# Three dense matmuls ahead of each level of the first stage of a recurrent-attention and MLP kernel

## The chip, the cores and the metric

One core of a Trainium2 chip runs the kernel. The metric is the device time of one execution in microseconds; the lower the better. Before the change it is 1013.24 us, the median of three runs (1012.25 to 1013.42).

## The reference

Everything is float32. A linear recurrence over 768 steps (4 batches, 8 heads, 48 channels a head) is followed by an RMS norm, a gated MLP (384 to 1536 to 384) and a squared-ReLU MLP (384 to 2048 to 384), over 3072 tokens.

```python
for t in range(S):
    cur = einsum('bhd,bhe->bhde', u[None] * k[t], v[t])
    y[t] = einsum('bhd,bhde->bhe', r[t], state + cur)
    state = w[t][..., None] * state + einsum('bhd,bhe->bhde', k[t], v[t])
xn = y / sqrt(mean(y * y) + 1e-6) * rms_g
x = (silu(xn @ w_gate) * (xn @ w_val)) @ w_out
out = (s * relu(x @ w_in) ** 2 + b) @ w_out2
```

## The kernel before

The 3072 tokens are worked in six stages (`NSB`) of 512. A stage is two blocks (`blk` 0 and 1) of 256 tokens. The first program block, `attention_and_gated_phase`, does the recurrence and the gated MLP; a second one does the squared MLP. From stage 1 on, the recurrence of stage s is interleaved with the gated MLP of stage s-1, so that TensorE always has 512-column matmuls beside the small ones. Stage 0 has nothing to be interleaved with: `first_attention` does it alone, and only then does the first gate matmul (L609) start.

The recurrence is done by doubling. At level l (0 to 6) the queries R in the second half of each pair of 2^l tokens are matched against the keys K. `level(s, l, blk)` issues 32 float32 matmuls on a 64 x 64 quarter of the array each, 32 columns wide, which the trace shows as 64 weight loads and 64 matmuls (L481). When they are done, VectorE multiplies K by the decays of that level (L923), copies the tile under a mask from PSUM to `near` (`place`, L940, levels 0 to 4) and doubles the decays (L915); GpSimd multiplies R by the decays (L1189). The next level of the same block waits for K and R. Level 5 is placed by ScalarE (L734), level 6 is `top_level` (L499), placed by ScalarE too (L752). In what follows (l, blk) is a level of stage 0.

Stage 0 runs by the list `FIRST_ORDER`: (0,0), (1,0), (0,1), (2,0), (1,1), (3,0), (2,1), (4,0), (3,1), (5,0), (4,1), (6,0), (5,1), (6,1). All engines follow their own program in order. The tiles of stage 0 are two banks each (the program's names in brackets): block 0 alternates between `level_ps` and `mix_gate_ps`, block 1 between `o01_ps` (o_ps in the trace) and `value_o2_ps` (value_o_ps), by whether l is even or odd. So a level must wait, in `level_out`, for level l-2 of its own block to be placed.

TensorE also runs matmuls whose results nobody reads. `run_up(15)` does 15 of 128 x 128 x 128 on a tile of ones (`y_sb[0]`) at the start. `keep_busy(n, ps)` does n of the same shape on the identity; it stands ahead of level (4,1), after (6,0), (5,1) and (6,1), and at some later places. Each such float32 matmul shows as two weight loads and two matmuls.

SyncE issues the loads of stage 0 by what TensorE has finished: three pieces of the gated weights (`w_raw`, 384 KB each) after (0,1), keys and queries by token after (1,0) and (1,1), values and one weight piece each after (2,0) and (2,1), the sixth weight piece after (3,1). ScalarE copies the first six weight pieces (`upper_weights`, L785) in order, each when it has landed, before it places level (5,0); level (6,0) waits for that placement.

Of the kernel before, what the change touches and what calls it, by code (L numbers as in the profile page):

```python
# [14 lines left out]
P = 128  # L15
# [10 lines left out]
NEAR = LV - 2  # L26
# [25 lines left out]
def wait(eng, sem, value):  # L52

    if not isinstance(value, int) or value > 0:
        eng.wait_ge(sem, value)
# [58 lines left out]
def placed(s, l, blk):  # L114

    return FIRST_PLACED.index((l, blk)) + 1 if s == 0 else 2 * NEAR + (NEAR - 1) * (s - 1) + l


def copied(s, blk):

    return 2 * (blk + 1) if s == 0 else 2 * (s + 2)
# [22 lines left out]
def attention_and_gated_phase(nc, block, a, whole, first, x1_dram, y_dram, x1_out, x_hi, x_lo, const_in_squared, level_ps, mix_gate_ps,  # L144
# [38 lines left out]
    with ExitStack() as ctx:  # L183
        def sb(name, shape, dt=F32):
            return ctx.enter_context(nc.sbuf_tensor(name, shape, dt, side="right"))
# [10 lines left out]
        y_sb = [sb(f"y{i}", [P, DM]) for i in range(CH)]  # L196
# [49 lines left out]
    def level_tile(s, l, blk):  # L246

        if s > 0:
            return pairs_ps(s, blk)[:, :, blk * HALF:(blk + 1) * HALF]
        ps = ((level_ps, mix_gate_ps), (o01_ps, value_o2_ps))[blk][l % 2]  # L250
        return ps[:].rearrange("p (j t) -> p j t", t=SUB)[:, :, 0:HALF]
# [42 lines left out]
    def level_out(eng, s, l, blk):  # L294

        if l < 0:
            return
        if l < NEAR:
            wait(eng, cp_done, placed(s, l, blk))
        else:  # L300
            wait(eng, near_done, copied(s, blk))

    def keys_ready(eng, s, l, blk):
        if l == 0:
            eng.wait_ge(k_in[blk], (s + 1) * 16)
        else:
            wait(eng, kmul_done, level_no(s, l - 1, blk))

    def queries_ready(eng, s, l, blk):
        if l == 0:  # L310
            eng.wait_ge(r_in[blk], (s + 1) * 16)
        else:
            wait(eng, rmul_done, level_no(s, l - 1, blk))
# [15 lines left out]
    def halves(ap, l):  # L329

        return ap.rearrange("p (n two m) -> p n two m", two=2, m=1 << l)
# [131 lines left out]

    @block.tensor
    def _(pe):
        def level(s, l, blk):
            if s == 0:
                level_out(pe, s, l - 2, blk)
            elif l > 1:
                level_out(pe, s, l - 1, blk)  # L470
            if s > 0 and l == 1:
                wait(pe, yo_done, CH * s)
            keys_ready(pe, s, l, blk)
            queries_ready(pe, s, l, blk)
            keys = HALF if l == NEAR else SUB
            for q in range(Q):
                for i in range(2):
                    for h in range(2):
                        rows = slice(h * SUB, (h + 1) * SUB)
                        first_key = q * P + i * SUB  # L480
                        mm = pe.matmul(level_tile(s, l, blk)[i * SUB:i * SUB + keys, h * Q + q],  # L481
                                       K[blk][rows, first_key:first_key + keys],
                                       halves(R[blk][rows, first_key:first_key + SUB], l)[:, :, 1],
                                       start=True, stop=True, skip_group_check=True)
            mm.then_inc(level_done, 1)
# [155 lines left out]
        def attention(s, k):  # L641
            if k in LEVEL_AT:
                for blk in range(2):
                    level(s, LEVEL_AT.index(k) + 1, blk)
            if k == TOP_AT:
                for blk in range(2):
                    top_level(s, blk)
            if k == 20:
                turn_keys(s, 0)
                turn_keys(s, 1)  # L650
                turn_keys(s, 2)
            if k == 22:
                turn_keys(s, 3)
                update(s, 0)
                update(s, 1)
            if k == 24:
                update(s, 2)
                update(s, 3)
                attend(s, 0)
            if k == 26:  # L660
                attend(s, 1)
# [7 lines left out]
        def first_attention():  # L669

            run_up(15)
            for l, blk in FIRST_ORDER:
                if l == LV - 1:
                    top_level(0, blk)
                    level_out(pe, 0, NEAR - 2 if blk == 0 else NEAR, 1)
                    keep_busy(2, value_ps)
                else:
                    level(0, l, blk)
                if l == NEAR - 1 and blk == 0:
                    pe.wait_ge(eye_in, 16)  # L680
                if (l, blk) == (NEAR, 0):
                    level_out(pe, 0, NEAR - 3, 1)
                    keep_busy(1, o01_ps)
                if (l, blk) == (NEAR, 1):
                    level_out(pe, 0, NEAR, 0)
                    keep_busy(1, mix_ps)
                if (l, blk) == (NEAR, 1):
                    turn_keys(0, 0)
                    turn_keys(0, 1)
# [893 lines left out]
```

## Time and profile before

| What | Value |
|---|---|
| median of 3 runs | 1013.24 us |
| the profiled execution's own time | 1013.42 us |
| its span, first to last instruction | 1011.3 us |
| mean granted TensorE clock | 0.985 of full |
| TensorE matmul busy | 994.9 us (98%) |
| VectorE busy | 537.8 us (53%) |
| ScalarE busy | 323.6 us (32%) |
| GpSimd busy | 268.5 us (27%) |
| first gate matmul (end of stage 0's recurrence) | starts at 60.06 us |

Times in the trace are counted from the first instruction, so the execution's own time is 2.1 us more than the span. A matmul counts as busy from its start to a modelled end, so matmuls that follow each other closely overlap in the rows: the start of the next group says more than the length of one. The granted clock has two levels, 1.00 for 2.4 GHz and 0.50 for 1.2 GHz.

### The profile page before, as it was taken

The numbers are of one execution on the slowest core, as the hardware profiler recorded it, in microseconds if no ns is written. First come the engines' busy times: TensorE is split into PE (matmuls) and PEld (weight loads), VectorE is DVE, ScalarE is ACT, GpSimd is POOL, SyncE is SP. The second block draws the span as 40 slices with busy tenths as digits, with TensorE's granted clock in tenths as the row PEclk, the third lists the DMA queues.
The fourth block names the chain that finished last, engine by engine and source line by source line (L and its number), as shares of the span: only waits on it lengthen the run. The fifth ranks groups of instructions, "written<-read, shape, count | busy, mean of one in ns | idle before, by whom it ended". The sixth has DMA issues, their size and how long they took to land.

```text
span 1011.3 us, 24572 instructions
## 1 busy us (share of the span) xinstructions
PE 994.9 (98%) x10584; PEld 862.9 (85%) x10584; DVE 537.8 (53%) x723; ACT 323.6 (32%) x550; POOL 268.5 (27%) x189
## 2 busy tenths in 40 slices
PE   7889999999999999999999999999999999999998
PEld 6878888888888888888888888998998989989898
DVE  6799857764676577557743225506226054161440
ACT  1442323233222313231323445406235053161340
POOL 4655723552463166216700650000000000000000
PEclk7799999999999999999999999999999999999999
DMA  7380252116013501440126201010010010100000
GB/s 273 118 327 5 90 165 93 49 51 217 33 49 111 188 3 52 155 141 3 48 61 232 69 16 64 9 39 16 16 48 0 23 39 8 54 0 16 16 8 23
DMA packets 41980, 73.99 MB, mean 73 GB/s; under 512 B 19105, under 2 KB 26273, under 8 KB 40609
## 3 DMA queue, kind: packets, MB, share of 16 engines
q1 hardware_dynamic: 41312, 71.52, 20.9%
q8 instruction: 73, 1.20, 0.5%
q10 hardware_dynamic: 576, 1.13, 0.3%
q14 instruction: 19, 0.15, 0.0%
HBM read 59.27 MB, written 13.37 MB: 72 GB/s over the span
## 4 chain that ended last, share of the span: by engine, by line
PE 87%; DVE 1%; issue 0%; ACT 0%; DVEq 0%
PE value_o_ps L609 13%; PE mix_gate_ps L609 13%; PE o_ps L1404 10%; PE level_ps L47 10%; PE o_ps L621 9%; PE mix_gate_ps L1404 5%; PE value_o_ps L1404 5%; PE mix_gate_ps L47 5%; PE value_o_ps L47 5%; PE value_o_ps L621 4%; PE level_ps L481 4%; PE mix_gate_ps L557 2%; PE level_ps L557 2%; PE level_ps L535 1%; PE level_ps L499 0%; PE level_ps L519 0%
## 5 line engine op out<-in xcount | busy, mean ns | idle before, releaser
L1478 DVE SCALAR_TENSOR_TENSOR sqr<-relu,sb_col 128x512 f32<-128x512 f32 x96 | 72.3, 753 | 216.9 <-ACT relu L1436 216.9
L1189 POOL TENSOR_TENSOR R<-R,arena 128x512 f32<-128x512 f32 x72 | 117.5, 1649 | 187.2 <-PE level_ps L481 161.9
L1057 DVE TENSOR_TENSOR u_raw<-value_o_ps,u_raw 128x512 f32<-128x512 f32 x66 | 45.5, 689 | 110.8 <-PE value_o_ps L609 110.8
L806 ACT ACTIVATE u_raw<-mix_gate_ps 128x512 f32<-128x512 f32 x72 | 43.1, 598 | 182.8 <-PE mix_gate_ps L609 182.7
L813 ACT ACTIVATE u_hi<-u_raw 128x512 fp32r<-128x512 f32 x66 | 41.7, 631 | 152.3 <-DVE u_raw L1057 152.3
L609 PE MATMUL value_o_ps<-x_hi,w_hi 128*128 128x512 f32 x216 | 85.1, 394 | 0.0
L609 PE MATMUL mix_gate_ps<-x_hi,w_hi 128*128 128x512 f32 x216 | 84.7, 392 | 0.0
L609 PE MATMUL value_o_ps<-x_hi,w_lo 128*128 128x512 f32 x216 | 84.1, 389 | 0.0
L609 PE MATMUL mix_gate_ps<-x_hi,w_lo 128*128 128x512 f32 x216 | 84.1, 389 | 0.0
L609 PE MATMUL mix_gate_ps<-x_lo,w_hi 128*128 128x512 f32 x216 | 84.1, 389 | 0.0
L609 PE MATMUL value_o_ps<-x_lo,w_hi 128*128 128x512 f32 x216 | 84.1, 389 | 0.0
L923 DVE TENSOR_TENSOR K<-K,arena 128x512 f32<-128x512 f32 x72 | 70.2, 989 | 22.3 <-PE level_ps L481 12.8
L1065 DVE TENSOR_TENSOR u_lo<-u_raw,u_hi 128x512 fp32r<-128x512 f32 x66 | 73.0, 1106 | 12.5 <-ACT u_hi L813 12.1
L1483 DVE SCALAR_TENSOR_TENSOR g_lo<-sqr,sb_col,g_hi 128x512 fp32r<-128x512 f32 x96 | 71.5, 745 | 0.8
L1427 ACT ACTIVATE g_hi<-sqr,sb_col 128x512 fp32r<-128x512 f32 x96 | 68.8, 716 | 1.3 <-DVE sqr L1478 1.3
L1404 PE MATMUL o_ps<-wt_hi,g_hi 128*128 128x384 f32 x192 | 64.1, 334 | 0.0
L1404 PE MATMUL o_ps<-wt_lo,g_hi 128*128 128x384 f32 x192 | 64.1, 334 | 0.0
L1404 PE MATMUL o_ps<-wt_hi,g_lo 128*128 128x384 f32 x192 | 64.1, 334 | 0.0
L621 PE MATMUL o_ps<-u_hi,wo_hi 128*128 128x512 f32 x144 | 60.3, 419 | 0.0
L481 PEld LDWEIGHTS level_ps<-R,K 64*64 64x64 f32 (+1 forms) x3392 | 50.1, 133 | 8.9 <-issue 8.8
L621 PE MATMUL o_ps<-u_hi,wo_lo 128*128 128x512 f32 x144 | 56.5, 392 | 0.0
L621 PE MATMUL o_ps<-u_lo,wo_hi 128*128 128x512 f32 x144 | 56.4, 392 | 0.0
(190 smaller groups left out, 2309.4 us busy)
## 6 DMA issues: line engine op xcount, KB each, us to landing
kr_nat<-kr SPq DMA_DIRECT2D x10, 1152.0 KB, 5.7
K<-kT SPq DMA_DIRECT2D x12, 512.0 KB, 4.5
arena<-wT SPq DMA_DIRECT2D x12, 512.0 KB, 6.4
R<-rT SPq DMA_DIRECT2D x10, 512.0 KB, 4.2
w_raw<-wgv SPq DMA_DIRECT2D x12, 384.0 KB, 5.2
v_sb<-v SPq DMA_DIRECT2D x12, 384.0 KB, 4.1
x_scratch<-x_sb SPq DMA_DIRECT2D x18, 256.0 KB, 2.3
x_raw<-x_scratch SPq DMA_DIRECT2D x6, 768.0 KB, 4.3
```

The lines of the kernel that those rows point to most:

```text
L47: mm = pe.matmul(ps, w[:, cols], x[:, k], start=(k == 0 and w is win_hi and x is x_hi), stop=(k == KT - 1 and w is win_lo))
L481: mm = pe.matmul(level_tile(s, l, blk)[i * SUB:i * SUB + keys, h * Q + q], K[blk][rows, first_key:first_key + keys], halves(R[blk][rows, f ...
L609: mm = pe.matmul(ps[:], w[:, f, j, k], x[:, k], start=(k == 0 and w is w_hi and x is x_hi), stop=(k == KT - 1 and w is w_lo))
L621: mm = pe.matmul(o_ps[j][:], w[:, f, j * P:(j + 1) * P], x[:, f % 2], start=(f == 0 and w is wo_hi and x is u_hi), stop=(f == F1 - 1 and w ...
L923: dve.tensor_tensor(k, k, decay(blk, l, 1), ALU.mult).then_inc(kmul_done, 1)
L1057: dve.tensor_tensor(u[:, f % 2], value_ps[:], u[:, f % 2], ALU.mult).then_inc(u_done, 1)
L1065: dve.tensor_tensor(u_lo[:, f % 2], u[:, f % 2], u_hi[:, f % 2].bitcast(F32), ALU.subtract).then_inc(ulo_done, 1)
L1189: pool.tensor_tensor(q, q, decay(blk, l, 0), ALU.mult).then_inc(rmul_done, 1)
L1404: mm = pe.matmul(o_ps[t][:, 0:DM], g[:, f, t * P:(t + 1) * P], w[:, f], start=(f == 0 and g is g_hi and w is wt[0]), stop=(f == F2 - 1 and ...
L1427: act.activation(g_hi[:, f], sq[f % 2][:], ACT.Identity, bias=sb_col[:, 1:2]).then_inc(ghi_done[0], 1)
L1478: dve.scalar_tensor_tensor(out=sq[f % 2][:], in0=relu[f % 2][:], scalar=sb_col[:, 0:1], in1=relu[f % 2][:], op0=ALU.mult, op1=ALU.mult).th ...
L1483: dve.scalar_tensor_tensor(out=g_lo[:, f], in0=sq[f % 2][:], scalar=sb_col[:, 1:2], in1=g_hi[:, f].bitcast(F32), op0=ALU.add, op1=ALU.subt ...
```

## The change

`level` calls a new helper for levels 1 to 4 of both blocks of stage 0 (eight calls), after the wait for the tile to be free and ahead of the waits for keys and queries. The helper issues three matmuls of ones, 128 x 128 x 128, into the first 128 columns of the tile that the level writes next. The level's own matmuls overwrite those columns.

```diff
     @block.tensor
     def _(pe):
+        def stay_warm(ps):
+
+            for _ in range(3):
+                pe.matmul(ps[:, 0:P], y_sb[0][:, 0:P], y_sb[0][:, 0:P], start=True, stop=True, skip_group_check=True)
+
         def level(s, l, blk):
             if s == 0:
                 level_out(pe, s, l - 2, blk)
+                if 0 < l < NEAR:
+                    stay_warm(((level_ps, mix_gate_ps), (o01_ps, value_o2_ps))[blk][l % 2])
             elif l > 1:
                 level_out(pe, s, l - 1, blk)
```

## Rows read from the trace of the kernel before

**Rows 1.** The page: busy time of the engines, and the granted clock in 40 slices.
```profile
PE 994.9 (98%) x10584; PEld 862.9 (85%) x10584; DVE 537.8 (53%) x723; ACT 323.6 (32%) x550; POOL 268.5 (27%) x189
...
PEclk7799999999999999999999999999999999999999
```
**Rows 2.** Stretches: length, busy PE, PEld, DVE, ACT, POOL, clock, DMA share, GB/s.
```profile
6.50:12.00 5.50, 2.33 (x130) 2.08 (x128) 3.11 (x4) 0.00 (x0) 2.47 (x2) 1.00 0.84 315
12.10:20.50 8.40, 7.54 (x256) 7.20 (x256) 7.83 (x10) 1.89 (x3) 6.04 (x4) 0.50 0.65 213
...
34.10:39.30 5.20, 5.18 (x109) 4.78 (x110) 2.65 (x6) 2.63 (x5) 3.27 (x3) 0.50 0.49 151
...
60.00:300.00 240.00, 239.12 (x3593) 198.07 (x3593) 177.94 (x227) 68.94 (x117) 110.56 (x73) 1.00 0.30 104
```
**Rows 3.** Waits of TensorE, whole span: total us, times, longest.
```profile
PE mix_gate_ps L481 <- POOL R L1189: 2.4, 1, 2.4
...
PE o_ps L481 <- issue: 2.0, 2, 1.7
PE level_ps L499 <- ACT near L734: 1.7, 1, 1.7
```
**Rows 4.** Timeline of TensorE: start us, length us, then the idle time before in brackets.
```profile
10.11 1.14 PE L481 MATMUL mix_gate_ps<-R,K 64*64 64x32 f32 x64 [2.42 <-POOL R L1189]
12.04 1.93 PE L481 MATMUL o_ps<-R,K 64*64 64x32 f32 x64 [0.80 <-DMA R<-rT]
13.85 1.93 PE L481 MATMUL level_ps<-R,K 64*64 64x32 f32 x64
...
24.21 0.31 PE L481 MATMUL o_ps<-R,K 64*64 64x32 f32 x1 [1.67 <-issue]
...
26.62 1.93 PE L481 MATMUL value_o_ps<-R,K 64*64 64x32 f32 x64 [0.28 <-POOL R L1189]
...
34.12 1.13 PE L499 MATMUL level_ps<-R,K 64*64 64x64 f32 x32 [1.65 <-ACT near L734]
35.18 1.22 PE L639 MATMUL value_o_ps<-eye 128*128 128x128 f32 x4
36.33 1.08 PE L481 MATMUL value_o_ps<-R,K 64*32 64x32 f32 x64
...
37.92 1.75 PE L519 MATMUL mix_gate_ps<-eye,K 128*128 128x128 f32 x8
39.60 0.69 PE L499 MATMUL o_ps<-R,K 64*64 64x64 f32 x32
...
44.68 1.16 PE L639 MATMUL value_o_ps<-eye 128*128 128x128 f32 x8
```
**Rows 5.** Timeline of VectorE: the key multiplies of (2,0), (1,1) and (3,0).
```profile
16.66 1.64 DVE L923 TENSOR_TENSOR K<-K,arena 128x512 f32<-128x512 f32 x1
...
19.84 0.68 DVE L923 TENSOR_TENSOR K<-K,arena 128x512 f32<-128x512 f32 x1
...
21.91 0.68 DVE L923 TENSOR_TENSOR K<-K,arena 128x512 f32<-128x512 f32 x1
```
**Rows 6.** Timeline of GpSimd's query multiplies: (2,1) and (4,0); then (5,1).
```profile
24.80 2.78 POOL L1189 TENSOR_TENSOR R<-R,arena 128x512 f32<-128x512 f32 x2 [3.18 <-PE o_ps L481]
...
37.61 1.57 POOL L1189 TENSOR_TENSOR R<-R,arena 128x512 f32<-128x512 f32 x1 [0.60 <-PE value_o_ps L481]
```
**Rows 7.** Timelines of SyncE's queue and of ScalarE around the sixth weight piece.
```profile
28.60 4.24 SPq L388 DMA_DIRECT2D w_raw<-wgv  x3
...
32.13 0.84 ACT L785 ACTIVATE w_hi<-w_raw 128x768 fp32r<-128x768 f32 x1 [1.61 <-DMA w_raw<-wgv]
32.88 1.18 ACT L734 ACTIVATE near<-mix_gate_ps 32x512 f32<-32x512 f32 x2
```
**Rows 8.** DMA queues in 14.5 to 15.0 and 21.75 to 22.0: packets, MB, share.
```profile
q8 instruction: 1, 0.02, 19.0%
...
q8 instruction: 1, 0.02, 23.7%
```

## The prediction

> **What bounds the kernel now.** I read the page first, then the stretches, then TensorE's waits, then the timelines of the first 60 us. The page says that TensorE is busy for 98% of the span, with the clock below full only in the first two of 40 slices [rows 1]. From 60 us on the stretches show TensorE busy for 239.12 of 240.00 us at full clock [rows 2]; nothing of the change lies there, so that whatever moves the first gate matmul (60.06 us) moves the end by as much. All that is at stake is stage 0's recurrence.
>
> There TensorE is busy too, but slow: it has the full clock in 6.5 to 12.0 us and half of it in 12.1 to 39.3 us [rows 2]. A level's 64 matmuls take 1.14 us at 2.4 GHz and 1.93 us at 1.2 GHz [rows 4]. Ahead of the fall TensorE had idled 2.42 us for R, done one level, and idled 0.80 us for a load [rows 4]. Ahead of the rise it did level (5,1), one `keep_busy` matmul and eight full-width transposes back to back from 37.92 us [rows 4]. So the quarter-array levels did not bring the clock back in 27 us, although they keep the busy column nearly full (7.54 of 8.40 us); full-width work did.
>
> A faster TensorE is worth only what the waits leave. Four things stand behind it:
> - VectorE, busy 7.83 of 8.40 us in 12.1 to 20.5 us [rows 2]. The key multiply of (2,0) starts at 16.66 us, though that level ended at 13.85 + 1.93 = 15.78 us; those of (1,1) and (3,0), at 19.84 and 21.91 us, have no idle time before them either [rows 4, 5]. Up to 23 us VectorE is some 0.9 us or more behind TensorE and sets the pace.
> - A gap of 1.67 us before the last matmul of (2,1), at 24.21 us, put down to issue [rows 3, 4]. VectorE and GpSimd then wait too: GpSimd idles 3.18 us [rows 6]. At 21.75 us the instruction queue moved one block of 16 KB (0.02 MB) [rows 8].
> - The chain from (3,1), whose end is 26.62 + 1.93 = 28.55 us: SyncE issues the sixth weight piece at 28.60 us, it has landed at 32.13 us, ScalarE copies it for 0.84 us, places (5,0) for 1.18 us, and only then does (6,0) start, at 34.12 us, after TensorE has idled 1.65 us [rows 4, 7]. This is 5.57 us in which TensorE's clock does not matter.
> - From 34.12 to 39.60 us TensorE sets the pace at half clock [rows 2, 4].
>
> **The change, part by part.** It removes nothing, adds no wait and moves no DMA directly. It adds 8 x 3 = 24 matmuls, 48 weight loads and 48 matmul records. Price at 1.2 GHz: eight full-width records from 37.92 to 39.60 us are 0.21 us each; the four of `keep_busy` from 35.18 to the next start at 36.33 us are 0.29 us each, the change to small tiles included [rows 4]. A set of six records costs 1.26 to 1.73 us; I take 1.5. At 2.4 GHz: eight in 1.16 us, 0.145 each, is the dear end [rows 4], half of 0.21 the cheap one: 0.63 to 0.87 us a set; I take 0.8, near the row measured at that clock. A full level and its set are then 1.03 + 0.8 = 1.8 us at full clock, about what the level alone costs now (starts 12.04 and 13.85 us: 1.81 us). That is the whole bargain: with the clock up the sets are paid by the faster levels, with the clock low they come on top.
>
> *The set ahead of (1,0)* falls in the idle 2.42 us before 10.11 us [rows 4] and costs nothing. If that cover were gone it would cost 0.8 us. It ends near 8.4 us, so that TensorE idles again before (1,0) and before (0,1); I expect the clock to fall at about 12 us all the same.
>
> *The set ahead of (2,0)* is therefore run at low clock and delays (2,0) by about 1.5 us, to an end near 16.6 us if the clock rises during it. VectorE takes up that level at 16.66 us anyway [rows 5]. Cost 0; without that cover, 0.8 to 1.7 us.
>
> *The sets ahead of (1,1), (3,0), (2,1)*, at full clock: (1,1) ends near 18.4 us and (3,0) near 20.4 us; VectorE takes them at 19.84 and 21.91 us [rows 5]. Cost 0, gain 0: here the change buys nothing, because VectorE is late. If they ran at low clock, they would cost 1.5 us each less that lag.
>
> *The gap at 24.21 us.* One block of instructions was moved at 14.5 and the next at 21.75 us [rows 8], and two levels are 2 x 128 records, so a block holds about two levels. The five sets up to (2,1) put 60 records ahead of the place where TensorE ran out, so that the same block is needed about half a level earlier, and is asked for earlier, ahead of the 768 KB load that SyncE issues after (1,1). The DMA engines are 0.65 busy in 12.1 to 20.5 us [rows 2]. The bounds: the gap stays as it is (0), or goes (-1.7 us). I take the middle, -0.9 us, since nothing in the trace says which. The Trainium skill, page "Runtime: NRT & Kernel Launch", section "Instruction fetch mechanics", says that blocks are 16 KiB or 256 instructions and that crossing into a new one is mostly hidden. The trace disagrees with "hidden" here, with 1.67 us of idle; by that rule the gap would be something else and would stay, and the sum below would be -0.8 instead of -1.7 us.
>
> *The sets ahead of (4,0) and (3,1).* (3,1) waits for R of (2,1), which GpSimd begins at 24.80 us, right after (2,1), and needs some 1.4 us for [rows 6]; (4,0) and the set ahead of (3,1) fit into that at full clock (1.1 + 0.8 us) but for a few tenths. Faster level against set: 0 (bounds -0.3 and +0.6 us). At low clock they cost 1.5 us each.
>
> *The sixth weight piece* then comes as much earlier as (3,1) ends, 0.9 us; *the set ahead of (4,1)* lies in the 1.65 us of idle before (6,0) and is free [rows 4].
>
> *The tail, 34.12 to 39.60 us.* With the clock up, (6,0), two `keep_busy` matmuls, (5,1) and the transposes would take half of 5.5 us, but (6,1) needs R of (5,1), and GpSimd has to do that of (6,0) first, 1.57 us each [rows 6]: 34.8 + 2 x 1.57 + 0.4 for the hand-overs = 38.3 us against 39.60, a gain of 1.3 us. If the idle before (6,0) lets the clock fall first, it is nothing. I take -0.8 us, the larger part, since the added set fills some of the idle.
>
> Sum: 0 + 0 + 0 - 0.9 + 0 - 0.8 = -1.7 us against the profiled execution's 1013.42 us: 1011.7 us. That execution lies 0.2 us above the median of 1013.24 us, so against the median I say 1011.5 us.
>
> **The rivals.**
> *The clock stays low (slower).* For it: six sets cannot help before the clock has risen, a third to a half of TensorE's time would still be quarter-array levels, and the 0.85 us of `keep_busy` beside (6,0) did not raise it [rows 4]. Against it: the transposes at 37.92 us did, after 1.4 us of themselves and one more matmul [rows 4], and a set of 1.3 us every 3.3 us is nearer to that. The price: from 12.04 us TensorE sets the pace, seven levels at 1.81 us spacing and six sets of 1.5 us: (3,1) ends at 12.04 + 6 x 1.81 + 1.93 + 9.0 = 33.8 us instead of 28.55 us. That is +5.3 us (3.8 to 6.7 for sets of 1.26 to 1.73 us), and the weight piece hands it on: 1018.5 us. It decides if the clock is still low at about 19 us; from there VectorE's lag is used up.
>
> *The clock rises and falls again.* The gap near 22 to 24 us is idle after two rather sparse levels. If the clock falls there, the sets ahead of (4,0) and (3,1) cost 1.5 us each, with about 1 us of it hidden: +2 us, 1015.2 us. For it: at 12 us it fell after such a pattern. Against it: the sets thin the idle out.
>
> *The clock rises and all moves.* The gap goes whole and the clock holds to the end of the tail: -1.7 - 1.3 = -3.0 us, 1010.2 us. The DMA engines speak against it: 0.65 busy on the mean while those weights load [rows 2].
>
> *It doesn't matter:* the gap stays and the tail is cold, 1013.2 us. For it: VectorE, the load of the weights and the gap each bound a part of their own.
>
> **How the numbers follow.** Chances: forecast (a part of the gap, a part of the tail, 1010.9 to 1012.6 us) 0.34; stays low 0.32; falls again 0.13; all moves 0.09; doesn't matter 0.12. The likeliest gives 1011.5 us. A measurement of this kernel can tell 0.2%, 2.0 us, from no change: faster is below 1011.2 us, slower above 1015.3 us. Faster: 0.09 and half of the forecast's 0.34, 0.26, and a little for a price of the sets near its cheap end: 0.29. Slower: 0.32 and half of 0.13, 0.38, and 0.03 for cases with the gap grown: 0.41. The rest, 0.30, is the same. The range is 1010.0 to 1019.0 us, since the two large cases lie on both sides; the likeliest one's own is 1010.9 to 1012.6 us.
>
> **What would show it.** Right: granted clock 1.00 from about 15 to 19 us, level rows of 1.14 us from there, VectorE's key multiplies of (2,0), (1,1), (3,0) within 0.3 us of 16.66, 19.84 and 21.91 us, (2,1) ending before 24.0 us, (6,0) starting at 33.2 us, the first gate matmul near 58.4 us. Wrong: clock 0.50 beyond 19 us and levels about 3.3 us apart; (6,0) after 37 us. Wrong as well if the clock never falls at 12 us, or if the gap before 24.21 us is still 1.7 us long.

## The result, and the profile after

| | before | after |
|---|---|---|
| median, 9 runs each | 1013.42 us | 1019.05 us |
| lowest to highest | 1012.25 to 1014.94 us | 1015.20 to 1021.25 us |
| ratio | | 1.0053 (95%: 1.0043 to 1.0062) |
| profiled execution | 1013.42 us, span 1011.3 | 1018.00 us, span 1015.9 |
| first gate matmul starts | 60.06 us | 64.34 us |

The change makes the kernel 0.53% slower, 5.4 us. The forecast was 1011.5 us; the measured time is nearest to that of the rival "the clock stays low", 1018.5 us.

The stretches of the changed kernel, with the columns of [rows 2], answer to the rows there:

```profile
6.50:12.00 5.50, 3.20 (x135) 2.85 (x134) 3.04 (x4) 0.00 (x0) 2.39 (x2) 0.99 0.85 324
12.10:20.50 8.40, 8.40 (x197) 7.82 (x200) 6.01 (x9) 2.28 (x3) 4.92 (x3) 0.50 0.63 216
...
34.10:39.30 5.20, 5.20 (x160) 4.85 (x154) 3.30 (x5) 1.38 (x3) 2.63 (x2) 0.51 0.50 154
...
56.50:59.80 3.30, 1.71 (x49) 1.47 (x41) 3.16 (x6) 2.14 (x8) 2.21 (x4) 1.00 0.52 148
60.80:64.10 3.30, 2.42 (x18) 2.00 (x18) 2.52 (x7) 2.08 (x6) 1.93 (x2) 1.00 1.00 287
```

The kernel before, with its transposes of y in 56.5 to 59.8 us:

```profile
56.50:59.80 3.30, 3.30 (x18) 3.25 (x16) 2.28 (x6) 2.08 (x6) 1.51 (x1) 0.50 1.02 396
```

In 12.1 to 20.5 us TensorE is now busy all the time (8.40 us, 7.54 before), at the same half clock, while VectorE has gone from 7.83 to 6.01 us [rows 2]. The pace has passed from VectorE to TensorE. A fuller busy column did not bring the clock back here.

The timeline of TensorE in the changed kernel, with the columns of [rows 4]. L469 is the added helper:

```profile
12.10 1.93 PE L488 MATMUL o_ps<-R,K 64*64 64x32 f32 x64 [0.78 <-DMA R<-rT]
13.96 1.65 PE L469 MATMUL level_ps<-y 128*128 128x128 f32 x6
15.54 1.94 PE L488 MATMUL level_ps<-R,K 64*64 64x32 f32 x64
17.40 1.65 PE L469 MATMUL value_o_ps<-y 128*128 128x128 f32 x6
18.98 1.93 PE L488 MATMUL value_o_ps<-R,K 64*64 64x32 f32 x64
...
32.74 1.93 PE L488 MATMUL value_o_ps<-R,K 64*64 64x32 f32 x64
...
39.88 0.69 PE L506 MATMUL level_ps<-R,K 64*64 64x64 f32 x32 [0.42 <-ACT near L741]
...
44.58 0.69 PE L506 MATMUL o_ps<-R,K 64*64 64x64 f32 x32 [0.58 <-DVE K L930]
```

No row from 12.10 us to (3,1) at 32.74 us waits for anything. A set goes from 13.96 to 15.54 us, 1.58 us; a level from 15.54 to 17.40 us, 1.86 us. Six of each are 20.64 us, and 12.10 + 20.64 is 32.74 us: that accounts for the whole stretch. Before, (0,1) to (3,1) took 26.62 - 12.04 = 14.58 us [rows 4], of which six levels were 11.16 us and the rest, 3.42 us, was waiting. So the sets added 6 x 1.58 = 9.48 us, the waits hid 3.42 us of it, the gap of 1.67 us at 24.21 us included, and (3,1) ends 6.1 us later.

VectorE's key multiplies of (2,0), (1,1) and (3,0), which answer to [rows 5], now wait for TensorE:

```profile
17.64 0.69 DVE L930 TENSOR_TENSOR K<-K,arena 128x512 f32<-128x512 f32 x1 [0.84 <-PE level_ps L488]
...
21.08 0.69 DVE L930 TENSOR_TENSOR K<-K,arena 128x512 f32<-128x512 f32 x1 [1.58 <-PE value_o_ps L488]
...
24.52 0.69 DVE L930 TENSOR_TENSOR K<-K,arena 128x512 f32<-128x512 f32 x1 [1.30 <-PE mix_gate_ps L488]
```

From (3,1) the weight piece hands the delay on, as in [rows 7]: ScalarE's copy of the sixth piece and the placement of (5,0) in the changed kernel:

```profile
37.90 0.84 ACT L792 ACTIVATE w_hi<-w_raw 128x768 fp32r<-128x768 f32 x1 [5.20 <-DMA w_raw<-wgv]
38.65 1.18 ACT L741 ACTIVATE near<-mix_gate_ps 32x512 f32<-32x512 f32 x2
```

(6,0) starts at 39.88 us, 5.76 us later than before. From there a part is given back. The clock is up from 39.2 us on, so (6,0) to (6,1) takes 4.70 us instead of 5.48 us. It is also up during the transposes of y, in 60.8 to 64.1 us, where the kernel before did them at 0.50, so (6,1) to the first gate matmul takes 19.76 us instead of 20.46 us. 5.76 - 0.78 - 0.70 = 4.28 us, the shift of the gate matmul; the span grew by 4.6 us. From the gate matmul to the end of the span it is 951.2 us before and 951.6 us after: nearly all of the loss lies ahead of the gate matmul. The medians are 5.6 us apart, because the profiled execution of the change is among its quicker ones. Its nine runs have mean clocks of 0.982 to 0.992, and the quickest (1015.2 us) is the one of 0.992. That suggests that the clock came back earlier in that run, but it has no profile.

### The profile page after: what moved, and what is told of

The parts are those of the page before. It is cut to its first block, busy times and chain, and to the rows that moved or that the text cites. A ratio compares the mean times of both kernels' runs of the same rounds, so it can differ in the third digit from the quotient of the medians.

```text
span 1015.9 us, 24668 instructions
## 1 busy us (share of the span) xinstructions
PE 1002.6 (99%) x10632; PEld 869.3 (86%) x10632; DVE 536.8 (53%) x723; ACT 323.6 (32%) x550; POOL 269.4 (27%) x189
## 4 chain that ended last, share of the span: by engine, by line
PE 87%; DVE 1%; issue 0%; ACT 0%; DVEq 0%
PE value_o_ps L616 13%; PE mix_gate_ps L616 13%; PE o_ps L1411 10%; PE level_ps L47 10%; PE o_ps L628 9%; PE mix_gate_ps L1411 5%; PE value_o_ps L1411 5%; PE mix_gate_ps L47 5%; PE value_o_ps L47 5%; PE value_o_ps L628 4%; PE level_ps L488 4%; PE mix_gate_ps L564 2%; PE level_ps L564 2%; PE level_ps L542 1%; PE level_ps L506 0%; PE level_ps L526 0%
## 5 line engine op out<-in xcount | busy, mean ns | idle before, releaser
L1072 DVE TENSOR_TENSOR u_lo<-u_raw,u_hi 128x512 fp32r<-128x512 f32 x66 | 73.8, 1119 | 12.5 <-ACT u_hi L820 12.1
L628 PE MATMUL o_ps<-u_hi,wo_lo 128*128 128x512 f32 x144 | 56.5, 392 | 0.0
```

The source lines that it names most:

```text
L628: mm = pe.matmul(o_ps[j][:], w[:, f, j * P:(j + 1) * P], x[:, f % 2], start=(f == 0 and w is wo_hi and x is u_hi), stop=(f == F1 - 1 and w ...
L1072: dve.tensor_tensor(u_lo[:, f % 2], u[:, f % 2], u_hi[:, f % 2].bitcast(F32), ALU.subtract).then_inc(ulo_done, 1)
```

## The experiments

The kernels with added matmuls take the number of matmuls of a set from a table, `stay_warm(ONES.get((l, blk), 0), tile)`; e11, e12 and e15 add none, and e9 is the change itself. The diffs are shortened and give the table; the change would be 3 for levels 1 to 4, both blocks. Each matmul makes four records in TensorE's stream, two weight loads and two matmuls, of which the timelines show the matmuls. "Before" in a ratio is the kernel before, run on the same chip beside it (median 1013.25 to 1014.03 us there).

### The free set, and the clock held up from the start

```diff
 # e1_first_set_only
+ONES = {(1, 0): 3}
 # e3_fill_and_sets
+ONES = {the change, but (1, 0): 10, and (0, 1): 3}
 # e4_fill_only
+ONES = {(1, 0): 10, (0, 1): 3}
 # e6_kick_then_sets
+ONES = {the change, but (2, 0): 9}
```

> Only the set of three ahead of (1,0), in TensorE's idle time; the other seven sets are out. Theory (the sets run at half clock come on top, one after the other): this one costs nothing, 1013.4 us, within 1 us of the kernel before; the clock still falls near 12 us. Rival (24 more matmuls shift the instruction blocks, and that costs): a shift of 12 records already moves the time by 1 us or more, and the 1.67 us gap near 24 us changes.

> The idle time before (1,0) and (0,1) is filled with 10 and 3 matmuls of ones, and the seven later sets of three stay. Theory: the clock does not fall near 12 us and the sets hold it, the levels take 1.14 us, a set 0.7 to 0.8 us, and the whole is 1 to 3 us faster than before, 1010.5 to 1012.5 us. Rival (the sets cost by themselves, whatever the clock): about as slow as the change, 1016 to 1019 us, with the clock up. Second rival: the clock falls at 12 us or soon after all the same; then as the change.

> The same fill of 10 and 3 matmuls in the idle time before (1,0) and (0,1), and no set after it. Theory: the clock falls later than 12 us but falls, since the levels alone do not hold it; 0 to 1.5 us faster than before, 1012 to 1013.5 us. Rival (the levels hold the clock once it is up): clock full to the end of the stage, 2 us or more faster, 1011 us or less, and faster than with the sets.

> The change with nine matmuls ahead of (2,0) instead of three, so that TensorE does only full-width work for 3.8 us at half clock. Theory: the clock rises within or right after them, the later sets are then cheap and hold it: dearer than the fill by the 2 to 2.5 us by which (2,0) is late, 1013 to 1015 us, faster than the change by 3 to 5 us. Rival (the sets cost whatever the clock): slower than the change by up to 2.5 us, 1020 us or more. Second rival: the clock rises and falls again, 1016 to 1019 us.

| kernel | median | ratio to before (95%) | gate matmul in the profile |
|---|---|---|---|
| e1_first_set_only | 1013.13 us | 0.9992 (0.9983 to 1.0001) | 60.42 us |
| e3_fill_and_sets | 1016.03 us | 1.0021 (1.0012 to 1.0030) | 61.80 us |
| e4_fill_only | 1022.58 us | 1.0092 (1.0076 to 1.0108) | 60.52 us |
| e6_kick_then_sets | 1014.90 us | 1.0011 (0.9998 to 1.0024) | 60.30 us |

The first set is free, as forecast. The kick came out as expected, and 4 us faster than the change. The two fills did not: 1016.0 us against 1010.5 to 1012.5 us expected with the sets, 1022.6 us against 1012 to 1013.5 us without. The three tell what a set does at either clock. In the kick, TensorE does eighteen full-width records in a row at half clock; then everything is at full clock:

```profile
14.00 4.21 PE L471 MATMUL level_ps<-y 128*128 128x128 f32 x18
18.14 1.25 PE L489 MATMUL level_ps<-R,K 64*64 64x32 f32 x64
19.32 0.94 PE L471 MATMUL value_o_ps<-y 128*128 128x128 f32 x6
20.19 1.14 PE L489 MATMUL value_o_ps<-R,K 64*64 64x32 f32 x64
21.25 0.94 PE L471 MATMUL mix_gate_ps<-y 128*128 128x128 f32 x6
```

A set and a level are 21.25 - 19.32 = 1.93 us here, against 3.44 us in the changed kernel with the same instructions. The clock holds until 35.5 us, past two gaps of 0.79 and 1.01 us, and falls behind a third, of 0.98 us ahead of (6,0). The gate matmul starts within 0.3 us of before, although (2,0) began 4.3 us late. So the rival "a set costs whatever the clock" is out: the price of a level with its set, which the forecast took at 1.8 us, was near, and the clock was missing.

In the fill with sets the clock does not fall at 12 us; the pace is again 1.93 us. Then TensorE runs out of instructions within (2,1):

```profile
19.59 0.94 PE L471 MATMUL o_ps<-y 128*128 128x128 f32 x6
20.45 0.42 PE L489 MATMUL o_ps<-R,K 64*64 64x32 f32 x12
23.46 1.71 PE L489 MATMUL o_ps<-R,K 64*64 64x32 f32 x52 [2.59 <-issue]
25.10 1.65 PE L471 MATMUL level_ps<-y 128*128 128x128 f32 x6
26.68 1.93 PE L489 MATMUL level_ps<-R,K 64*64 64x32 f32 x64
```

The clock falls at 22.8 us, within those 2.59 us, and the later sets cost 1.58 us each. Of the 3.6 us that this profile is slower than before, 1.7 us are there at the gate matmul and the rest behind it, with 0.9 us in two gaps put down to issue. This is the rival "rises and falls again", seen in a kernel in which the clock had been up. In the fill without sets it falls earlier, at 18.9 us, with TensorE idle for 1.40 us and 0.82 us beside the levels: with the sets it held there. Whether by their full-width work or by the idle time that they fill is not told apart. But that kernel is 9 us slower than before with a gate matmul only 0.5 us later. Something behind stage 0 costs more than all of this; the third group of experiments is about that.

### How the cost goes with the number of matmuls

```diff
 # e2_one_each
+ONES = {1 for levels 1 to 4, both blocks}
 # e5_six_each
+ONES = {6 for levels 1 to 4, both blocks}
 # e8_tiny_sets: the change, each matmul cut to 64 rows, 64 columns, 32 moving
+pe.matmul(ps[0:SUB, 0:HALF], y_sb[0][0:SUB, 0:SUB], y_sb[0][0:SUB, 0:HALF], ...)
 # e10_late_sets_only
+ONES = {(2, 1): 3, (4, 0): 3, (3, 1): 3, (4, 1): 3}
```

> One matmul of ones ahead of each of the eight levels instead of three. Theory (array time at half clock, 0.21 us a record and 0.3 us a set for the change of tile size): a set costs 0.7 us instead of 1.6, VectorE's lag and the gap near 24 us hide most, (3,1) ends at 29 to 30 us and the kernel is 0.5 to 2 us slower than before (1014.5 to 1016 us). Rival (what a set costs is its place between two levels, not its length): more than half of the change's cost, 1017 us or more with (3,1) ending after 32 us.

> Six matmuls of ones ahead of each level instead of three. Nine in one place raised the clock in an earlier run, three per level did not. Theory (the more full-width work there is beside the levels, the earlier the clock comes back): it rises by 20 us, a set then costs 1.4 us, TensorE paces at 2.5 us a level, (3,1) ends at 29.5 to 32 us: slower than before by 1 to 4 us, yet not slower than the change. Rival (only an unbroken stretch raises it): it stays low, sets of 2.9 us, (3,1) ends at about 42 us, 12 us or more slower than before.

> The change with each of its 24 matmuls cut to 64 rows, 64 columns of weights and 32 columns of ones: the same number of instructions at the same places, with next to no array time (a level's own matmuls are spaced 0.03 us a record, so a set is 0.2 us). Theory (the change costs by the time of full-width matmuls at half clock): VectorE's lag and the idle times hide it, within 1.5 us of before, and (3,1) ends before 29.5 us. Rival (96 more instructions move the blocks in which they are fetched): the larger part of the 5 us stays, or gaps put down to issue appear later in the kernel.

> Only the four later sets of three, ahead of (2,1), (4,0), (3,1) and (4,1); none ahead of (1,0), (2,0), (1,1), (3,0). Theory (sum of half-clock sets, less what was idle): the set ahead of (2,1) costs up to 1.6 us less the wait for K, those ahead of (4,0) and (3,1) 1.6 us each less 0.3 us, the one ahead of (4,1) nothing: 2.5 to 4 us slower than before, (6,0) at 36.6 to 38 us. Rival (what counts is that TensorE paces from 12 us on): the three early sets carry as much as the late ones, so this half costs only half of 5 us or less, under 2.5 us.

> The change itself once more, for the spread of its runs (1015.2 to 1021.25 us against 1012.25 to 1014.94 us of before) and a second profile. Theory: the clock stays low through the sets in the profile too, or rises at different places from run to run, which makes the spread; median 1018 to 1020 us. Rival (the spread comes from gaps in the supply of instructions behind stage 0): the rows behind 64 us show gaps put down to issue of 1 us or more in the slower executions.

| kernel | median | ratio to before (95%) | end of (3,1) |
|---|---|---|---|
| e8_tiny_sets | 1014.74 us | 1.0015 (1.0006 to 1.0025) | 28.9 us |
| e2_one_each | 1015.12 us | 1.0023 (1.0013 to 1.0033) | 29.8 us |
| the change again (e9) | 1019.15 us | 1.0058 (1.0044 to 1.0072) | 34.7 us |
| e5_six_each | 1020.87 us | 1.0061 (1.0043 to 1.0080) | 34.7 us |
| e10_late_sets_only | 1019.39 us | 1.0056 (1.0042 to 1.0070) | 31.5 us |

The same number of added instructions at the same places, with next to no array time, costs 1 to 1.5 us; one full-width matmul a set costs 2.3 us; three cost 5.4 to 5.9 us. The tiny sets and one each came out as expected. In the profile of one each, a set is 0.73 us (14.23 to 14.96 us) and a level 1.86 us, and the waits still hide most. At the end of (3,1) the delay follows the array time at half clock less 3.4 us of waiting: 6 x 0.73 - 3.4 = 1.0 us for one each, where 1.3 us was measured, and 6.1 us for three each, as measured. It rises steeply once that cover is used up.

Six each missed its expectation of 1 to 4 us slower. The clock did come back, but at 23.6 us and not by 20 us. The timeline, within (1,1) and the set behind it:

```profile
19.32 2.93 PE L471 MATMUL value_o_ps<-y 128*128 128x128 f32 x12
22.18 1.76 PE L489 MATMUL value_o_ps<-R,K 64*64 64x32 f32 x64
23.87 1.60 PE L471 MATMUL mix_gate_ps<-y 128*128 128x128 f32 x12
25.41 1.13 PE L489 MATMUL mix_gate_ps<-R,K 64*64 64x32 f32 x64
```

By then two sets of 2.86 us had been paid, and a set is 1.54 us even at full clock. (3,1) ends as late as in the changed kernel. Behind its gate matmul, at 64.78 us, this kernel also has four gaps put down to issue, 2.0 us together, so that its time is not array time alone.

The change again gave the same picture: clock at half until 39.2 us, the gate matmul at 64.30 us, no gap of 1 us or more behind 64 us. The expected rival for the spread of the runs, gaps in the slower executions, finds no support in either profile; but both profiles are of quicker executions, so it is not ruled out, and the spread is not explained.

The late sets moved the gate matmul by only 0.8 us (60.89 us, in an execution in which the first level began 0.5 us late and the clock rose at 33.7 us, within the last set), yet the kernel is as slow as the whole change, where 2.5 to 4 us were expected. As in the fill without sets, the loss lies behind stage 0.

### The place of the instruction blocks

```diff
 # e13_shift_52: 13 small matmuls (as in e8) ahead of (1,0), nothing else
+ONES = {(1, 0): 13}
 # e17_shift_96: 12 of them ahead of (1,0), 12 ahead of the first transposes of y
+ONES = {(1, 0): 12}
...
             keep_busy(4, gate_ps)
+            for _ in range(12):
+                pe.matmul(gate_ps[0:SUB, 0:HALF], eye[0:SUB, 0:SUB], eye[0:SUB, 0:HALF], ...)
             first_turn(range(0, C))
```

> Thirteen small matmuls of ones (64 x 64 x 32) ahead of (1,0) alone, in TensorE's idle 2.1 us, and no set anywhere else: 52 records more and no array time where it counts. The fill (52 more) and the late sets (48 more) lost 4 to 6 us behind stage 0 in gaps put down to issue. Theory (the place of the instruction blocks decides these gaps): this kernel is 4 us or more slower than before, 1017 us or more, with gaps behind 50 us, and stage 0 ends as before (60 to 61 us). Rival (the gaps came from the other timing of loads or from the clock): within 1.5 us of before.

> Twelve small matmuls (64 x 64 x 32) ahead of (1,0) and twelve behind the last keep_busy before the first transposes of y, both in idle time of TensorE: as many records as the change adds, 96, and no full-width work. Theory (the change costs by half-clock array time; a shift of 96 records is a harmless one): within 1.5 us of before. Rival (the shift carries a good part of the 5.6 us): 2 us or more slower than before, with gaps put down to issue behind 60 us.

| kernel | records added | median | ratio to before (95%) |
|---|---|---|---|
| e13_shift_52 | 52 | 1021.48 us | 1.0081 (1.0066 to 1.0096) |
| e17_shift_96 | 96 | 1014.19 us | 1.0006 (0.9998 to 1.0015) |

Thirteen small matmuls in idle time, 1.7 us long where TensorE waited 2.4 us anyway, make the kernel 8 us slower, more than the change. Stage 0 ends as before (gate matmul 59.91 us). From the gate matmul to the end of the span it is 955.5 us here, 958.5 us with the late sets and 957.3 us with the fill alone, against 951.2 us before. Both kernels here came out as expected. The waits of TensorE behind 60 us (total, times, longest), in the shift by 52, then in the late sets (48 records), then in the fill alone (52 records):

```profile
PE level_ps L565 <- issue: 3.8, 2, 2.0
```
```profile
PE value_o_ps L617 <- issue: 2.6, 1, 2.6
PE mix_gate_ps L565 <- issue: 1.5, 1, 1.5
```
```profile
PE level_ps L565 <- issue: 3.3, 2, 2.1
```

Neither kernel of the main comparison has such a row there. In all three the larger gaps lie near 235 and 335 us, in or next to `attend`, whose matmuls are short and many. Each of these six gaps ends about 2 to 2.8 us after the instruction queue moved a block: in the shift by 52, moves in 231.5 to 232.0 and 330.0 to 330.5 us, TensorE going on at 234.19 and 332.81 us. That fits a block used up before the next one has come; why the block came late there is not shown. The Trainium skill, page "Runtime: NRT & Kernel Launch", section "Instruction fetch mechanics", calls the cost of a 16 KiB boundary mostly hidden; the 3.8 us say that here it depends on where the boundary falls. Kernels with 48 and 52 records more are slow, those with 12, 32 and 96 more are not.

In the profile of the shift by 52 the gaps, 3.8 us and one of 0.2 us, are nearly the whole loss of 4.1 us. It was the quickest of its six (1017.51 us); the slowest, 1024.99 us, has a mean clock of 0.978 against 0.984 and no profile. What can come on top is seen in the two other kernels: behind the gap the clock is at half, from 235.1 to 241.9 us with the late sets and from 237.4 to 240.8 us in the fill alone, under 512-column matmuls. The late sets have six matmuls in 238 to 240 us, where the kernel before has ten (TensorE's busy time, then clock, DMA share and GB/s):

```profile
238.00:240.00 2.00, 2.00 (x6) 0.50 0.23 52
```

A shift of 96 records by itself costs 0.6 us most likely, 1.5 us at most, by its interval. So of the change's 5.4 us some 4 to 5 us are array time at half clock.

### The two bounds that TensorE's clock does not touch

```diff
 # e12_loads_later
-            sp.wait_ge(level_done, level_no(0, 1, blk))
-            load_natural(blk)
...
             sp.wait_ge(level_done, level_no(0, 3, 1) + f - 5)
             load_weights(f)
+            if f < 7:
+                load_natural(f - 5)
 # e11_place_first
-            for f in range(6):
+            for f in range(5):
                 upper_weights(f)
             place_near(0, [0])
             place_far(0, [0])
+            upper_weights(5)
 # e15_both: the two;  e16_both_fill_sets: the two and e3's table
```

> The kernel before, with the two 768 KB loads of keys and queries by token issued behind (3,1) and (5,0) instead of behind (1,0) and (1,1). Theory (the 1.67 us gap ahead of the last matmul of (2,1) is a block of instructions that queues behind these loads): the gap is under 0.3 us and (2,1) ends at 22.6 to 23 us; the sixth weight piece does not land later than its issue plus 3.5 to 6 us; 0 to 2 us faster than before. Rival (the gap has nothing to do with the load of the DMA engines): the gap is still there near 22.5 us.

> The kernel before with one edit: ScalarE copies the sixth weight piece behind the placement of (5,0) and (6,0) instead of ahead of it. Theory ((6,0) at 34.12 us hangs on the landing of that piece and not on TensorE's clock): (6,0) starts at 32.5 to 33 us right behind (4,1), and the kernel is 1 to 1.8 us faster, 1011.9 to 1012.7 us. Rival (something else is as late, such as the copy of K or R for (5,1)): under 0.5 us.

> The kernel before with both edits, the later loads by token and the placement ahead of the sixth piece; no ones beyond the run-up. Theory: no gap near 24 us, (6,0) at 32.5 to 33 us in a profile whose first level starts at 6.6 us, 1.5 to 3 us faster than before, 1010.8 to 1012.3 us. Rival (the two are the same microseconds): no faster than the better of the two.

> Both edits, with the fill of 10 and 3 and the sets of three: with the gap gone there is no idle time of 2.6 us in which the clock fell with the fill and the sets. Theory (sets are free where the clock is up, and the clock holds without the gap): clock full from 0 to 40 us, (6,0) at 30 to 32 us, 2 to 5 us faster than before, 1008.5 to 1011.5 us. Rival (136 more records bring gaps behind stage 0 that eat it): the end of stage 0 is 2 us or more earlier, the whole is not.

| kernel | median | ratio to before (95%) | (6,0) starts | gate matmul |
|---|---|---|---|---|
| e12_loads_later | 1013.23 us | 0.9992 (0.9983 to 1.0001) | 34.93 us | 60.11 us |
| e11_place_first | 1012.30 us | 0.9983 (0.9974 to 0.9992) | 32.94 us | 57.98 us |
| e15_both | 1012.18 us | 0.9989 (0.9978 to 1.0000) | 31.34 us | 57.09 us |
| e16_both_fill_sets | 1015.77 us | 1.0021 (1.0011 to 1.0031) | 35.14 us | 60.23 us |

With the later loads (2,1) runs through and (4,0) follows at once; the rows of TensorE in that kernel, where [rows 4] have the gap at 24.21 us:

```profile
21.80 1.94 PE L480 MATMUL o_ps<-R,K 64*64 64x32 f32 x64 [0.54 <-DVE K L922]
23.86 1.94 PE L480 MATMUL level_ps<-R,K 64*64 64x32 f32 x64
```

That supports the gap as a block held up behind the loads, in the kernel with its blocks where they were. But one profile a kernel is little here: with TensorE's stream unchanged the gap is 1.67 us in the kernel before and 2.49 us in e11. Nor did the kernel gain: (3,1) ends at 28.9 us, since smaller idle times of 0.54, 0.22 and 0.56 us came instead, in an execution whose first level began 0.6 us late. And the loads are not the whole of it: with the fill and the sets the same move of loads leaves a gap of 2.32 us at 20.9 us (before: 2.59 us). There the block was moved in 20.5 to 21.0 us, with the DMA engines 0.94 busy in the two microseconds ahead of it, and TensorE went on at 23.20 us; in the kernel before it was moved in 21.75 to 22.0 us and TensorE went on at 24.21 us. Weight pieces and values were still being loaded; that they were enough to hold the block up is argued, not shown. The expectation that the clock would hold to 40 us, and with it the 2 to 5 us of gain, failed: it fell at 23.8 us.

The placement ahead of the sixth piece did what it should: (6,0) follows (4,1) without a wait.

```profile
31.24 1.94 PE L481 MATMUL o_ps<-R,K 64*64 64x32 f32 x64 [0.26 <-POOL R L1190]
32.94 1.14 PE L499 MATMUL level_ps<-R,K 64*64 64x64 f32 x32
```

It is 0.17% faster than the kernel before, as expected, and is the best of all kernels here by its interval; it adds no matmul. Of the 2.1 us at its gate matmul, 1.2 us are the earlier (6,0); most of the rest comes from the transposes of y, done at full clock here too. Both edits together bring the gate matmul 3 us forward but are not clearly faster than the one, so that the expected 1.5 to 3 us are not borne out.

This kernel also has a row that bears on the forecast. TensorE does not idle ahead of (6,0), and the clock is up before the transposes:

```profile
36.10:36.60 0.50, 0.50 (x15) 0.30 (x3) 0.50 (x2) 0.36 (x2) 0.18 (x1) 1.00 0.86 344
...
36.14 0.49 PE L639 MATMUL mix_gate_ps<-eye 128*128 128x128 f32 x2
36.60 1.09 PE L519 MATMUL mix_gate_ps<-eye,K 128*128 128x128 f32 x8
```

Until then it had done (6,0), four records of `keep_busy` and (5,1). With both edits the clock rises 0.3 us into the transposes (35.4 us, transposes from 35.16 us). So the rise does not need the transposes that stood ahead of it in the kernel before.

## Why the prediction was wrong

- *The set ahead of (1,0) is free, and the clock falls at about 12 us all the same:* right (1.60 us of idle time left ahead of (1,0), clock 0.50 from 12 us, e1 within 0.1%).
- *The clock rises during the set ahead of (2,0):* wrong, and this is the step that failed. It stayed at 0.50 through all six sets, to 39.2 us, in both profiles of the change. All that the forecast says of full-clock sets hangs on it. Six records between two levels did not bring it back, twelve did after the second set, eighteen in a row did at once; with the late sets the clock rose at 33.7 us, within the first eight in a row, two of `keep_busy` and a set. The trace of before held the rise behind eight transposes and a `keep_busy`; I took that as enough for sets that have a level of 1.86 us between them. The reading itself was weak: in e11 the clock was back 0.5 us before the transposes began. What exactly brings the clock back stays open. The forecast had a chance of 0.34 against 0.32 for the clock staying low, so it was a guess at nearly even odds.
- *Price of a set:* 1.5 us forecast, 1.58 measured at half clock; 0.8 us against 0.87 (19.32 to 20.19 us in the kick) at full clock.
- *Cost 0 for the sets ahead of (2,0), (1,1), (3,0):* right only for the VectorE lag: 3.42 us of waiting did hide that much of 9.48 us.
- *The gap at 24.21 us goes in part:* in the changed kernel it went whole, presumably because TensorE was slower to use the blocks up. As a gain by itself it was not had: at full clock there are 2.59 us in the fill with sets and 0.79 and 1.01 us in the kick. The forecast's block of "about two levels" does not follow from the moves at 14.5 and 21.75 us, between which TensorE went through more than three levels; the next moves, in 25.0 to 25.5 and 29.0 to 29.5 us, are nearer to it.
- *The weight piece hands on what (3,1) loses:* right, 6.1 us there, 5.76 us at (6,0).
- *Tail -0.8 us:* -0.78 us, by luck. The forecast priced the tail at -1.3 us with the clock up and took -0.8 us between that and nothing; here the clock was up for all of it, and it gave only 0.78 us. (5,1) waits 0.19 us for R, the transposes wait 0.33 us and (6,1) 0.58 us for K from VectorE; the waits for K are not in the forecast's sum. Nor had I foreseen the further -0.70 us in the transposes of y.
- *The rival that held:* it gave +5.3 us; (3,1) at 33.8 us against 34.7 us measured, and missed the 1.48 us given back, the two partly cancelling.

What no part of the prediction had is the far side of an instruction shift: I looked for its effect only at 24.21 us, within stage 0. The change was lucky with its 96 records; the kernels with 48 and 52 more took 4 to 7 us more behind the gate matmul in their profiles.

## What to carry to other kernels

A dose of dense filler matmuls that does not bring the clock back is paid at half clock, less what waits hide. So look in the trace for what TensorE did ahead of each rise, in more than one kernel if you can, and try that much in one piece and in idle time before counting on it. Ask first what a faster TensorE would meet: here VectorE, a weight load and a ScalarE queue left 1 to 3 us to gain, and putting one ScalarE copy later gained more than any filler. And whenever instructions are added to a long unrolled stream, time the same number of near-empty ones in idle time beside it.

## What the runs showed of the hardware

- Fifty-two records more in TensorE's stream, in idle time, cost 8 us (1.0081); the profile has gaps of 1.8 and 2.0 us more than 220 us behind the edit. 12, 32 and 96 records more do not show such gaps.
- Between the move of an instruction block and TensorE's next instruction lay 2.2 to 2.7 us in two kernels (moved in 21.75 to 22.0 us, on at 24.21 us; in 20.5 to 21.0 us, on at 23.20 us).
- With the clock up, levels and sets at 1.93 us a pair held it for 10 and 16 us; levels alone, beside idle times of 1.40 and 0.82 us, lost it after 7 us; it was lost within a gap of 2.59 us, 2 us after the gap began.
- The clock came back to full with no transposes ahead of it (e11, 36.0 us), behind (6,0), four records of `keep_busy` and (5,1) without idle time; with 1.65 us of idle time ahead of the same work, in the kernel before, it came back at 39.4 us.
